# A fused attention, MLP and expert kernel: the router's logits of 15 row tiles as dot products on VectorE instead of transposes and matmuls on TensorE

## What is computed

```python
x = attention(q, k, v)                                  # (2304, 512)
xn = x / sqrt(mean(x * x) + 1e-6) * rms_g
y = (silu(xn @ w_gate) * (xn @ w_val)) @ w_out          # d_ff = 1536
logits = y @ router + modality_bias[modality_id]        # router: (512, 8)
e = argmax(logits); gate_w = softmax(logits)[e]
out = gate_w * (relu(y @ w1[e]) @ w2[e])                # w1[e]: (512, 1024)
```

## Time and profile before

| | us |
|---|---|
| median of 3 runs | 930.12 |
| lowest and highest | 929.95 to 930.21 |
| the profiled execution | 929.51 |
| its span | 927.7 |
| granted TensorE clock, mean | 0.984 |

### The profile page before, as it was taken

How to read it: one execution, slowest core, us unless ns; L and a number is a source line. 1 busy time by engine, 2 the same in 40 slices (tenths; PEclk the granted TensorE clock), 3 DMA queues, 4 the chain that set the end, 5 groups by cost and what they waited for, 6 DMA issues and landing times.

```text
span 927.7 us, 15901 instructions
## 1 busy us (share of the span) xinstructions
PE 898.6 (97%) x5433; PEld 767.6 (83%) x5433; DVE 456.4 (49%) x1239; ACT 360.9 (39%) x935; POOL 308.1 (33%) x366
## 2 busy tenths in 40 slices
PE   8989999999999999999999999999789999999996
PEld 5657898888878888799999999998678888888884
DVE  5864555433454345522433343774754466446651
ACT  5866413544444444421121131242243355335430
POOL 2734762344233342344234233240502222212221
PEclk9999999999999999999999999999889999999998
DMA  8972212222113211211121121610836355515521
GB/s 180 276 188 77 58 51 65 66 65 73 49 44 107 61 27 32 67 36 36 35 80 35 39 75 35 222 51 35 302 135 242 129 182 189 201 48 197 194 74 35
DMA packets 74486, 94.95 MB, mean 102 GB/s; under 512 B 38701, under 2 KB 42797, under 8 KB 74416
## 3 DMA queue, kind: packets, MB, share of 16 engines
q1 hardware_dynamic: 70656, 82.51, 29.2%
q0 software_dynamic: 3760, 11.54, 3.6%
HBM read 84.59 MB, written 10.22 MB: 102 GB/s over the span
## 4 chain that ended last, share of the span: by engine, by line
PE 90%; DVE 4%; ACT 1%; issue 1%; POOL 1%; DMA 1%; ACTq 0%; POOLq 0%; DVEq 0%
PE ps L1100 34%; PE ps L1139 15%; PE ps L1575 13%; PE ps L1590 11%; PE ps L1032 3%; PE ps L1061 2%; PE ps L1602 2%; PE ps L1042 2%; PE ps L1009 2%; PE ps L1166 1%; PE ps L1159 1%; PE ps L569 1%; PE ps L1150 1%; DMA xg<-x_rows,idx_gather 1%; DVE h_lo L1429 0%
## 5 line engine op out<-in xcount | busy, mean ns | idle before, releaser
L1418 DVE SCALAR_TENSOR_TENSOR h<-h,ps 128x384 f32<-128x384 f32 x72 | 39.9, 554 | 175.2 <-ACT h L1276 175.1
L906 POOL TENSOR_TENSOR sm<-sm,rinv 72x288 f32<-72x288 f32 (+1 forms) x51 | 45.6, 894 | 204.2 <-DVE rinv L1362 204.1
L1100 PE MATMUL ps<-x_hi,gate_hi 128*128 128x384 f32 x288 | 104.1, 362 | 0.0
L1100 PE MATMUL ps<-x_hi,val_hi 128*128 128x384 f32 x288 | 102.1, 354 | 0.0
L936 POOL CAST out_hi<-out_raw 128x512 fp32r<-128x512 f32 x72 | 46.6, 648 | 155.1 <-DMA out_raw<-in_moe_w_out 155.1
L1100 PE MATMUL ps<-x_hi,gate_lo 128*128 128x384 f32 x288 | 97.5, 338 | 0.0
L938 POOL TENSOR_TENSOR out_lo<-out_raw,out_hi 128x512 fp32r<-128x512 f32 x72 | 95.1, 1322 | 5.8
L1100 PE MATMUL ps<-x_hi,val_lo 128*128 128x384 f32 x288 | 96.9, 337 | 0.0
L1100 PE MATMUL ps<-x_lo,val_hi 128*128 128x384 f32 x288 | 96.9, 336 | 0.0
L1100 PE MATMUL ps<-x_lo,gate_hi 128*128 128x384 f32 x288 | 94.4, 338 | 0.0
L1139 PE MATMUL ps<-out_hi,h_hi 128*128 128x512 f32 x216 | 89.4, 414 | 2.1 <-DVE h_lo L1429 2.1
(11 more groups left out here) (248 smaller groups left out, 1926.2 us busy)
## 6 DMA issues: line engine op xcount, KB each, us to landing
w_raw<-in_moe_w SPq DMA_DIRECT2D x64, 512.0 KB, 6.6
out_raw<-in_moe_w_out SPq DMA_DIRECT2D x72, 256.0 KB, 2.6
x_rows<-y_tiles SPq DMA_DIRECT2D x18, 256.0 KB, 2.4
early_w_raw<-in_moe_w SPq DMA_DIRECT2D x8, 512.0 KB, 6.1
gate_raw<-in_moe_w_gate SPq DMA_DIRECT2D x4, 768.0 KB, 9.8
val_raw<-in_moe_w_val SPq DMA_DIRECT2D x4, 768.0 KB, 9.5
qk<-in_q SPq DMA_DIRECT2D x8, 288.0 KB
qk<-in_k SPq DMA_DIRECT2D x8, 288.0 KB
```

The lines of the kernel that those rows point to most:

```text
L906: pool.tensor_tensor(s3, s3, rinv[0:n, i, :].unsqueeze(2).to_broadcast([n, 4, c]), ALU.mult).then_inc(s_no, 1)
L1100: mm = pe.matmul(ps[:, bank, 0:CH], w[:, i, kk, cols], x[:, kk, :], start=(m == 0), stop=(m == n - 1))
L1418: dve.scalar_tensor_tensor(out=hf[n % 2][:, :], in0=hf[n % 2][:, :], scalar=1.0, in1=ps[:, 0, 0:CH], op0=ALU.add, op1=ALU.mult).then_inc(s ...
```

## The change

The logits of the 15 tiles of chunks 0 to 4 leave PE. `turn_y`, `logits` and ACT's `evac_yT` are gone, with their semaphores and their turns in bank 7. In their place:

- SP sends the whole router matrix to all partitions (`router_on_all`, 16 KB on each of 128 partitions, 2 MB written) at tick `ROUTER`, step 4 of chunk 3, when the last attention output is out. ACT copies it from there into eight contiguous rows `router_of_0` to `router_of_7`, each 128x512, one a tick from the last tick of step 4.
- SP loads tiles 0 to 8 of y back from DRAM into a ring of three (`y_again`), eight ticks ahead of their use. Tiles 9 to 14 are read from `y_tiles`, and ACT's `evac_y` of chunks 4 and 5 waits for their last use.
- DVE makes each logit as one `tensor_tensor_reduce` of 128x512 (`dot`), 8 for a tile, 120 in all. Each waits for the one before. Tiles 0 to 11 take one tick for a dot, from step 5 of chunk 3 to step 8 of chunk 4. Tiles 12 to 14 take three dots in two ticks, from sub 2 of step 0 of chunk 5 to sub 0 of step 3. `add_bias` now reads from SBUF.

`sm_early`, which had shared the space of `yT`, keeps that space.

```diff
@@ -112,17 +112,11 @@
-Y_TILE = {(c, t): at(c + 1, 3 + 2 * t, 2) if c < NC - 2 else at(c + 1, 1 + t, 0)
-          for c in range(NC - 1) for t in range(TT)}
-LOGITS = {k: s + 2 for k, s in Y_TILE.items()}
...
-         + [("y", k) for k in Y_AT.get(s, [])] + [("lg", k) for k in LOGITS_AT.get(s, [])]]
+         + [("ss", c) for c in SS_AT.get(s, []) if c] + [("rb", c) for c in SPREAD_AT.get(s, []) if c]]
@@ -137,6 +131,18 @@
+RELOADED = TT * (NC - 3)
+ROUTER = at(NC - 3, 4, 0)
+DOT = {(i, e): at(NC - 3, 5, 0) + E * i + e if i < TT * (NC - 2)
+       else at(NC - 1, 0, 2) + (E * (i - TT * (NC - 2)) + e) * 2 // 3
+       for i in range(TT * (NC - 1)) for e in range(E)}
+DOT_AT = by_tick((k, s) for k, s in DOT.items())
+DOTTED_AT = by_tick((i, DOT[i, E - 1] + 1) for i in range(TT * (NC - 1)))
+RELOAD_AT = by_tick((i, DOT[i, 0] - 8) for i in range(RELOADED))
+BY_EXPERT_AT = by_tick((e, DOT[0, e] - 1) for e in range(E))
@@ -307,6 +313,14 @@
+        ra = Region(xT_at + KT * 2 * S * 4)
+        rw_all = ra.put("router_on_all", [P, DM, E])
+        rw_of = [ra.put(f"router_of_{e}", [P, DM]) for e in range(E)]
+        y_again = [ra.put(f"y_again{i}", [P, DM]) for i in range(3)]
+        unread = ra.put("unread", [P, DM])
+        dots = ra.put("dots", [P, 2, E])
@@ -850,6 +865,15 @@
+                if s == ROUTER:
+                    sp.wait_ge(s_oe, G)
+                    sp.dma_start(rw_all[:, :, :].rearrange("p d e -> p (d e)"),
+                                 router_w.rearrange("d e -> (d e)").partition_broadcast(P)).then_inc(s_rwa, 16)
+                for i in RELOAD_AT.get(s, []):
+                    if i >= 3:
+                        sp.wait_ge(s_le, i - 2)
+                    sp.wait_ge(s_x2, 16 * TT * (i // TT + 1))
+                    sp.dma_start(y_again[i % 3][:, :], x2[i * P:(i + 1) * P, :]).then_inc(s_ya[i % 3], 16)
@@ -1140,25 +1160,6 @@
-            def turn_y(c, t):
...
-                for kk in range(KT):
-                    mm = pe.transpose(ps[:, 7, kk * P:(kk + 1) * P], ys[:, t, kk * P:(kk + 1) * P], ident[:, :])
-                mm.then_inc(s_yt, 1)
-
-            def logits(c, t):
...
-                pe.wait_ge(s_yte, TT * c + t + 1)
-                for kk in range(KT):
-                    mm = pe.matmul(ps[:, 7, 0:E], yT[:, kk, :], rw[:, kk, :],
-                                   start=(kk == 0), stop=(kk == KT - 1))
-                mm.then_inc(s_lg, 1)
@@ -1284,14 +1281,9 @@
-                    act.wait_ge(s_yt, TT * c)
+                if c > NC - 3:
+                    act.wait_ge(s_le, TT * c)
...
-            def evac_yT(c, t):
-
-                act.wait_ge(s_yt, TT * c + t + 1)
-                act.activation(yT[:, :, :].rearrange("p k n -> p (k n)"), ps[:, 7, :],
-                               ACT.Copy).then_inc(s_yte, 1)
@@ -1307,14 +1299,15 @@
+                for e in BY_EXPERT_AT.get(s, []):
+                    act.wait_ge(s_rwa, 16)
+                    act.activation(rw_of[e][:, :], rw_all[:, :, e], ACT.Copy).then_inc(s_rwe, 1)
@@ -1429,12 +1422,28 @@
-            def add_bias(c, t):
-                i = TT * c + t
+            def dot(i, e):
+
+                if e == 0 and i < RELOADED:
+                    dve.wait_ge(s_ya[i % 3], 16 * (i // 3) + 16)
+                if e == 0 and i >= RELOADED:
+                    dve.wait_ge(s_ye, i // TT + 1)
+                if i == 0:
+                    dve.wait_ge(s_rwe, e + 1)
+                if E * i + e:
+                    dve.wait_ge(s_dot, E * i + e)
+                if e == 0 and i >= 2:
+                    dve.wait_ge(s_le, i - 1)
+                y = y_again[i % 3][:, :] if i < RELOADED else ys[:, i % TT, :]
+                dve.tensor_tensor_reduce(out=unread[:, :], in0=y, in1=rw_of[e][:, :], scale=1.0, scalar=0.0,
+                                         op0=ALU.mult, op1=ALU.add,
+                                         accum_out=dots[:, i % 2, e:e + 1]).then_inc(s_dot, 1)
+
+            def add_bias(i):
                 if i == 0:
                     dve.wait_ge(s_bu, 6)
-                dve.wait_ge(s_lg, i + 1)
-                dve.tensor_tensor(logit[:, i, :], ps[:, 7, 0:E], bias_t[:, i, :], ALU.add).then_inc(s_le, 1)
+                dve.wait_ge(s_dot, E * i + E)
+                dve.tensor_tensor(logit[:, i, :], dots[:, i % 2, :], bias_t[:, i, :], ALU.add).then_inc(s_le, 1)
@@ -1458,8 +1467,10 @@
-                for key in LOGITS_AT.get(s, []):
-                    add_bias(*key)
+                for key in DOT_AT.get(s, []):
+                    dot(*key)
+                for i in DOTTED_AT.get(s, []):
+                    add_bias(i)
```

More of the change, by code:

```diff
@@ L222, in fused_kernel @@
         yT_at = res.at
-        yT = res.put("yT", [P, KT, P])
+        sm_early = res.put("sm_early", [P, 512])
         sq_at = res.at
@@ L244, in fused_kernel @@
         kT = [res.put(f"kT{i}", [P, WIN + S]) for i in range(2)]
-        sm = [res.put(f"sm{i}", [P, 512]) for i in range(SM - 1)] + [alias("sm_early", yT_at, [P, 512])]
+        sm = [res.put(f"sm{i}", [P, 512]) for i in range(SM - 1)] + [sm_early]
         pt = [res.put(f"pt{i}", [P, 4 * LQ]) for i in range(2)]
@@ L411, in fused_kernel @@
         s_bu = sem("bias_built")
-        s_yt = sem("y_tile_turned")
-        s_yte = sem("yT_evacuated")
-        s_lg = sem("logits_of_tile")
+        s_rwa = sem("router_on_all_loaded")
+        s_rwe = sem("router_by_expert")
+        s_ya = [sem(f"y_loaded_again{i}") for i in range(3)]
+        s_dot = sem("dot_products")
         s_le = sem("logits_read")
@@ L975, in bank_7_free @@
                     pe.wait_ge(s_nv, before[1] + 1)
-                elif before[0] == "rb":
+                else:
                     pe.wait_ge(s_xn, KT * before[1] + KT)
[L978 to L981, removed]
             def residues():
@@ L1142, in down @@
                     mm.then_inc(s_y, 1)
-            def turn_y(c, t):
-                if t == 0:
-                    pe.wait_ge(s_ye, c + 1)
-                bank_7_free(("y", (c, t)))
-                for kk in range(KT):
-                    mm = pe.transpose(ps[:, 7, kk * P:(kk + 1) * P], ys[:, t, kk * P:(kk + 1) * P], ident[:, :])
-                mm.then_inc(s_yt, 1)
-            def logits(c, t):
-                bank_7_free(("lg", (c, t)))
-                if c == 0 and t == 0:
-                    pe.wait_ge(s_small, 48)
-                pe.wait_ge(s_yte, TT * c + t + 1)
-                for kk in range(KT):
-                    mm = pe.matmul(ps[:, 7, 0:E], yT[:, kk, :], rw[:, kk, :],
-                                   start=(kk == 0), stop=(kk == KT - 1))
-                mm.then_inc(s_lg, 1)
             def keep_busy(n):
@@ L1192, in front_pe @@
                     spread_roots(c)
-                for key in Y_AT.get(s, []):
-                    turn_y(*key)
-                for key in LOGITS_AT.get(s, []):
-                    logits(*key)
                 if s == COUNT_1:
@@ L1309, in front_act @@
                         act.activation(dst, src, ACT.Copy).then_inc(s_qe, 1)
-                for key in Y_AT.get(s, []):
-                    evac_yT(*key)
                 if s == SPREAD[0] + 1:
```

3 lines of the change are left out of this document (removed).

## The result

| | before | after |
|---|---|---|
| median of the runs | 930.04 us | **940.09 us** |
| lowest to highest | 927.62 to 930.21, 4 runs | 935.4 to 946.38, 4 runs |
| profiled execution, span | 929.5 us, 927.7 us | 935.4 us, 933.6 us |
| mean granted clock | 0.984 | 0.987 |

The ratio is 1.0143, with a 95% interval of 1.0106 to 1.0181: **slower by 1.4%** (the two medians of the table alone give 1.0108, at the lower end of the interval).

A forecast was written before the change was run, and what follows sets the result against it. PE bounds the kernel, 6.27 us per MLP step; DVE becomes the bound where the dots land. -20.1 + 17.4 + 6.4 + 1.0 = +4.7 on 929.5 gives 934.2; the median lies 0.6 above, so 935, range 919 to 950.

The forecast's parts named there:

- What goes off PE, -20.1: Transposes, logits and slower up matmuls of fifteen tiles leave PE: 1.34 us a tile, 20.1 us less PE time.
- A dot, 0.61 to 0.725: Start-to-start time of a 128x512 dot on DVE: 0.61 us before another instruction, 0.725 before a dot; 0.67 taken.
- Blocking in the first stretch, 26 of at most 32.3: Chunk 3 step 5 to chunk 4 step 8: two-SBUF-input dots lose 26 us to POOL's reads; PE held up 17.4 us.
- DVE's other waits, 3.7: Unhidden DVE waits in the first stretch: h_lo 0.1 x 16, chunk's change 0.6, router's columns 1.5; 3.7 us.
- The clock: With all of it, microsecond pauses each step might lower TensorE's clock; three steps at half speed are of the same size.
- all of it: Rival, both stretches: dots of 0.725 us and blocking in full, +19.5, 950 us; chance 0.14.
- The second stretch, 6.4: 24 dots in 16 ticks in chunk 5: DVE needs 25.1 us, has 18.7; PE held up 6.4 us.
- The routing's lag, 1.0: Dense routing chain on DVE behind the second stretch lags: 0 to 2 us, 1.0 taken.
- At nothing: the reloads, ACT's room, the out blocks: Reloads of y, eight copies on ACT and out blocks cost nothing, if out blocks stay a step ahead.
- No blocking: Rival: dots' second input doesn't meet POOL; first stretch costs nothing, second 2.5 us; -17.6, 912.5 us; chance 0.13.
- Milder: Rival: half of the blocking, 16 and 2.4 us in the two stretches; -7.8, 922 us; chance 0.16, shared with Free links.
- Free links: Rival: waits between DVE instructions cost nothing, all dots 0.61 us; -2.5, 928 us; chance 0.16, shared with Milder.

The follow-up runs named there:

- Experiment 1: y_in_psum: the changed kernel, but ACT first copies each tile of y into PSUM, where the dots read it; 918.39 us, ratio 0.9905 to before.
- experiment 2: pool_reads_more: the changed kernel plus one POOL subtraction of 128x512 in each of the first stretch's 16 steps; 948.71 us, ratio 1.0213 to before.
- experiment 4: The changed kernel plus one POOL iota, which only writes SBUF, in each of the first stretch's 16 steps; 936.51 us, ratio 1.0102 to before.
- Experiment 6: last_tiles_on_pe: the changed kernel with the logits of tiles 12 to 14 back on PE; 931.96 us, ratio 1.0034 to before.
- Both forms of the kernel before: The unchanged kernel, 930.04 us, and the same with 16 more POOL subtractions of 128x512 in the first stretch, 926.85 us, ratio 0.9987.
- experiment 5: The changed kernel with two scratch rows, so each dot waits for the last but one; 932.2 us, ratio 1.0048 to before.

## Why the prediction was right, step by step

**The forecast** was 935 us and slower, by blocking; it came out slower, at 940.09, inside the range. The profiled execution it was reckoned against gave 935.4 where the sum said 934.2, but that agreement is luck: 2.8 us gained ahead of chunk 1 and 3.1 at the end, neither of them in the sum, against 7.0 us by which terms were too small (2.9, 0.7 and 3.4, below). The terms as measured add up to -20.1 + 20.3 + 7.1 + 4.4 = +11.7 and not to +4.7; the medians, 10 us apart, are nearer to that. One slip is in the recorded sum: 64.3 + 2.0 + 29.5 is 95.8 and not 96.3, so that its own terms give a hold-up of 16.9 and a time half a microsecond lower.

- **What goes off PE, -20.1:** right as far as it can be read. 9.4, 6.7 and 4.0 fall in the three places by the forecast's 1.34 a tile; the one stretch where nothing else changed, to chunk 3, step 5, measures 9.3 for seven tiles.
- **A dot, 0.61 to 0.725:** right; 0.62 and 0.73 in the rows above, 0.61 when unlinked.
- **Blocking in the first stretch, 26 of at most 32.3:** right in kind and size: 24.7, three quarters of full. Experiment 1 removes it and the time goes; experiments 2 and 4 show that it is POOL's reads. The same share came out for the work added in experiment 2. Of the signs named beforehand, the dots' mean (0.86 to 0.88) and the step (7.7 us) came as said; DVE's share did not, 93% and not above 95%, for the waits of the next item.
- **DVE's other waits, 3.7:** too small, and the largest part of why PE was held up 20.3 and not 17.4. From the stretch's start to the end of the scaling in step 9 (403.18 to 531.43) DVE took 128.3 us against 126.0, and that scaling ended 5.6 us after its gate product's start where the forecast had 3.3 + 3.0. DVE's idle time there is 8.4 us, some 1.5 of it links that the dot's figure already holds; 6.9 are waits. Two of them stand out. The router's columns cost 3.3 instead of 1.5. The load was as estimated (issued at 397.48, seen by ACT at 404.77, 7.3 us), but I had priced ACT's copies of the columns at nothing, and each lasted 1.25 us, three in a row 3.48:

```profile
404.77 3.48 ACT L1310 ACTIVATE router_of<-router_on_all 128x512 f32<-128x512 f32 x3 [2.29 <-DMA router_on_all<-in_moe_w_gate]
```

 The other is the chunk's change, priced at 0.6. There the two engines wait for each other in turn: PE stood 4.4 us for `h_lo` at 459.20, ran the down and gate products at the slower clock, and so DVE waited 2.8 us for the tanh of that gate product. The step took 14.8 us instead of 8.5.
- **The clock:** the prediction put its fall with the rival "all of it". It did fall, but briefly: after the 4.4 us pause nine down matmuls came 0.43 to 0.56 us apart instead of 0.23 and five gate ones 0.32 instead of 0.17, until 464.8, and the windows show 0.65 and 0.81 around them. That is 1.9 + 0.75 = 2.6 us of PE time, part of the 20.3; over the whole stretch the clock is 0.97.
- **The second stretch, 6.4:** 7.1 measured, with blocked time of 4.0 against 3.9.
- **The routing's lag, 1.0:** mis-sized; 4.4. I called the chain dense but didn't read its slack. In before, `hot_b` ends at 576.09 and PE takes it at 576.24: 0.15 us. After, the chain starts at 580.18, 1.6 us after the gate product that hides it, instead of 0.2 before it; and one of its steps, 0.22 long in before, lies beside POOL's subtraction of 581.01:

```profile
580.18 0.27 DVE L610 TENSOR_REDUCE top<-bias_then_logit 128x15 f32<-128x120 f32 x1
580.49 0.58 DVE L611 TENSOR_TENSOR bias_then_logit<-bias_then_logit,top 128x120 f32<-128x120 f32 x1
581.21 1.14 DVE L614 TENSOR_SCALAR pick<-bias_then_logit 128x120 f32<-128x120 f32 x1
...
583.33 0.22 DVE L620 CAST hot_b<-hot 128x120 bf16<-128x120 f32 x1
```
```profile
583.61 0.23 PE L667 MATMUL ps<-hot_b,upper 128*128 128x120 bf16 x1 [2.68 <-DVE hot_b L620]
...
585.23 0.53 PE L1120 MATMUL ps<-x_hi,val_hi 128*128 128x384 f32 x1
```

 PE waits 2.7 us, and then most of the matmuls behind it come 0.32 us apart instead of 0.17: the rest of that step takes 5.8 us instead of 4.3, another 1.5. y_in_psum has the same wait (2.8) and the same loss with hardly a dot blocked, so it is the dots' place just ahead of the chain, not blocked dots, that starts it: it starts 1.8 us later against the gate product, and is itself 1.2 longer, 3.4 us beside POOL's cast and subtraction instead of 2.2. Experiment 6 removes it.
- **At nothing: the reloads, ACT's room, the out blocks.** No wait of PE or DVE ends on a reload of y or on an out block in the two stretches, as said. ACT's copies were the one item at nothing that cost time.
- **Not in the sum: the end.** The part behind chunk 5, step 7, is 3.1 us shorter. There PE waits 0.3 us for the gathered rows instead of 1.9, and the clock in a 42 us piece some 84 us into it is 1.00 (686.00 to 728.00) instead of 0.92 (677.10 to 719.10). Two experiments tell these apart: last_tiles_on_pe waits 2.3 us for the gathered rows, longer than before does, and has the short end (331.4) with the clock at 1.00; pool_reads_more waits 0.3 and has a long one (333.7) with 0.92:

```profile
PE ps L591 <- DMA xg<-x_rows,idx_gather: 2.3, 1, 2.3
687.44:729.44 42.00, 40.06 (x191) 32.91 (x192) 25.54 (x28) 18.11 (x22) 6.84 (x10) 1.00 0.52 181
701.15:743.15 42.00, 40.24 (x181) 33.02 (x182) 24.04 (x27) 17.21 (x21) 5.63 (x8) 0.92 0.51 181
```

 So the short end goes with the clock of that piece and not with the gather. Both forms of the kernel before have the longer end (334.6, 335.0) and 0.92; the eight changed ones lie between 328.6 and 333.7, one of them at 0.92. Whether the change brings this is not shown, and why the clock differs stays open.

**The rivals.** *No blocking*, 912.5: its premise is refuted, but experiment 1 nearly realises it and gives 918.39. It is above the rival's figure, and what accounts for it is that 4.9 us of blocking are left and that PE is held up 3.3, 4.5 and 4.6 us in the three places, where the rival had 0, 2.5 and 0; the shorter end takes some of that back. *Milder*, 922, is refuted by the 24.7. *Free links*, 928, is refuted by the pitches, and by experiment 5: taking the links away changes the time. *All of it*, 950: three quarters, not all, and a clock that fell for microseconds, not for three steps.

## What to carry to other kernels

- An engine that is idle half the time isn't free for half a stretch of new work: before moving work to DVE, count what POOL reads in that stretch, and if the new instruction has two SBUF inputs, add about two thirds of POOL's busy time as a first guess (24.7 us for 38.2 here, in this one program). Moving one of the inputs to PSUM cost 0.59 us a tile on idle ACT and turned 1.4% slower into 1% faster.
- Read the slack where the bound engine takes a result, step by step: here it was 3.0 us in a plain step, less at a chunk's change, where even the lighter kernels wait, and 0.15 us at the routing chain. New work belongs in the first kind alone.
